# A fused linear-attention, Fourier and channel-mixing kernel: the gate computation in five parts issued in another order, zero matmuls placed elsewhere, Fourier tiles spread over more blocks

## The reference

```python
# stage 1, attention with a complex decay per token and channel
mag = np.sqrt(a_re * a_re + a_im * a_im)
scale = np.minimum(mag, 0.999) / (mag + 1e-06)
a_re_n, a_im_n = (a_re * scale, a_im * scale)
for t in range(S):
    new_re = ar * S_re - ai * S_im
    new_im = ar * S_im + ai * S_re
    kv = np.einsum('bhd,bhe->bhde', k[:, :, t], v[:, :, t])
    S_re, S_im = (new_re + kv, new_im)
    y[:, :, t] = np.einsum('bhd,bhde->bhe', q[:, :, t], S_re)
# stage 2
X = np.fft.fft(np.fft.fft(x, axis=1), axis=2)
u = x + np.real(X)
...
ch = np.maximum(un @ w_ch1, 0.0) @ w_ch2      # un is u, normalised by rows
return (u + ch)
# stage 3: token mixing and another two-layer product of the same sizes
```

## Time and profile before

| | us |
|---|---|
| runs | 1070.27, 1048.11, 1056.67 |
| median | 1056.67 |
| the profiled execution, own time | 1050.42 |
| its span (first to last instruction) | 1048.4 |
| PE busy | 982.1 (94%) |
| DVE busy | 514.9 (49%) |
| ACT busy | 357.8 (34%) |

### The profile page before, as it was taken

One profiled execution on the slowest core, in us unless ns is written; L12 is line 12 of the kernel. 1 busy time (PEld: TensorE's weight loads), 2 busy tenths in 40 slices (PEclk: granted clock), 3 DMA queues, 4 the chain that ended last, 5 costly groups with the idle time before them and its releaser, 6 DMA issues.

```text
span 1048.4 us, 15600 instructions
## 1 busy us (share of the span) xinstructions
PE 982.1 (94%) x6154; PEld 951.2 (91%) x6154; DVE 514.9 (49%) x940; ACT 357.8 (34%) x532; POOL 16.4 (2%) x12
## 2 busy tenths in 40 slices
PE   0389999999999999999999999999999999999997
PEld 0268889889899899999999999999999999999997
DVE  5888699999855654234324222542223214223220
ACT  7676666676531520220221221431213102121120
POOL 0000000000000000000000000030000000000000
PEclk9789899998999999999999999999999999999999
DMA  6689977986776064021021010010001001000000
GB/s 208 197 232 263 254 220 190 235 244 154 191 206 239 16 243 171 16 75 45 24 66 45 30 61 23 16 54 16 8 23 45 23 15 53 23 0 23 9 16 26
DMA packets 96745, 104.75 MB, mean 100 GB/s; under 512 B 13104, under 2 KB 90288, under 8 KB 96688
## 3 DMA queue, kind: packets, MB, share of 16 engines
q1 hardware_dynamic: 96688, 104.00, 33.6%
HBM read 70.86 MB, written 33.11 MB: 99 GB/s over the span
## 4 chain that ended last, share of the span: by engine, by line
PE 81%; DVE 8%; ACT 7%; issue 2%; DMA 0%; SPq 0%; DVEq 0%; ACTq 0%
PE bank L233 21%; PE bank L235 21%; PE bank L234 21%; PE bank L1173 3%; PE bank L1191 2%; DVE n_area L942 2%; PE bank L1189 2%; PE bank L1234 2%; PE bank L1250 2%; PE bank L1252 2%; PE bank L1202 2%; PE bank L1258 2%; PE bank L243 1%; DVE n_area L947 1%; DVE n_area L930 1%
## 5 line engine op out<-in xcount | busy, mean ns | idle before, releaser
L121 ACT ACTIVATE hh<-bank 128x384 fp32r<-128x384 f32 x192 | 94.5, 492 | 375.0 <-PE bank L235 375.0
L209 DVE SCALAR_TENSOR_TENSOR hl<-bank,hh 128x384 fp32r<-128x384 f32 x192 | 107.0, 557 | 195.6 <-ACT hh L121 195.6
L233 PE MATMUL bank<-w2h,hh 128*128 128x384 f32 x576 | 193.3, 336 | 0.0
L233 PE MATMUL bank<-nTh,w1h 128*128 128x384 f32 x576 | 193.0, 335 | 0.0
L235 PE MATMUL bank<-w2h,hl 128*128 128x384 f32 x576 | 192.5, 334 | 0.0
L234 PE MATMUL bank<-w2l,hh 128*128 128x384 f32 x576 | 192.5, 334 | 0.0
L235 PE MATMUL bank<-nTh,w1l 128*128 128x384 f32 x576 | 192.5, 334 | 0.0
L234 PE MATMUL bank<-nTl,w1h 128*128 128x384 f32 x576 | 192.4, 334 | 0.0
L233 PEld LDWEIGHTS bank<-nTh,w1h 128*128 128x128 f32 x576 | 108.1, 188 | 0.4 <-issue 0.2
L234 PEld LDWEIGHTS bank<-w2l,hh 128*128 128x128 f32 x576 | 108.2, 188 | 0.0
L234 PEld LDWEIGHTS bank<-nTl,w1h 128*128 128x128 f32 x576 | 108.1, 188 | 0.0
(11 more groups left out here) (156 smaller groups left out, 1294.1 us busy)
## 6 DMA issues: line engine op xcount, KB each, us to landing
w_area<-k_turn SPq DMA_DIRECT2D x24, 384.0 KB, 4.8
w_area<-q_turn SPq DMA_DIRECT2D x24, 384.0 KB, 6.1
q_turn<-w_raw SPq DMA_DIRECT2D x30, 192.0 KB, 3.0
k_turn<-n_area SPq DMA_DIRECT2D x24, 192.0 KB, 2.6
k_turn<-w_flat SPq DMA_DIRECT2D x24, 192.0 KB, 2.7
u_scratch<-h_area SPq DMA_DIRECT2D x24, 192.0 KB, 6.4
w_raw<-in_moe_w_ch SPq DMA_DIRECT2D x2, 2304.0 KB, 12.4
x_flat<-u_scratch SPq DMA_DIRECT2D x4, 1152.0 KB, 10.0
```

The costliest lines, as they stand in the source:

```text
L121: self.nc.scalar.activation(self.hh[:, m, :], self.mm_bank[(g * (KF + TPG) + m) % 2][:, 0:TG], ACT.Relu).then_inc(self.h_high, 1)
L209: self.nc.vector.scalar_tensor_tensor(out=self.hl[:, m, :], in0=self.mm_bank[(g * (KF + TPG) + m) % 2][:, 0:TG], scalar=0.0, in1=self.hh[: ...
L233: self.nc.tensor.matmul(out, lh, rh, start=(n == 0), stop=False)
```

## The change

- **Parts p0 to p4 are written out by hand**, interleaved with blocks 0 to 5 on ACT and DVE; the loop starts at block 6. `logs` is cut into `bounded` and `sums`, `magnitudes` loses its Abs to `moduli`, and `phases` is `half_turns`, `wrapped` per chunk, and `carried`. Counters `factored`, `summed`, `ended` and `qk_scaled` replace places in the running count of each part, so that the steps may stand in another order.
- **DVE issues `masked(0)` ahead of `phases(p2)`**, and `phases(p3)` is cut around `masked(3)`. ACT issues `keys_turned(0)` ahead of `inverses`, `arctangents` and `factors` of p2. There are six more table loads.
- **Zero matmuls**: 16, 2, 10, 1, 1, 8, 6, 5 in blocks 0 to 7, none in 12 and 18; 55 in all (60 before).
- **Fourier part**: `middle`, the width transforms and their evacuations move from j=1 to j=2. Tiles 0, 1 go to j=3, tile 2 to j=4, tile 3 to j=5, tiles 4 and 5 to j=0 and 1 of the batch after. For the last-but-one batch, tiles 4 and 5 run after block 23, in two other PSUM banks.
- **SP's queue**: block 0's products and `decay_back(p0)` go ahead of `decay_out(p1)`; `load_gates(p3)` follows at once, `load_qk(p3)` at the end of the opening.

```diff
 def transformed_at(...)
-            return {2: [0], 3: [1, 2], 4: [3, 4], 5: [5]}.get(j, [])
+            b, j = divmod(m, NCH)
+            n = b - 2 if j < 2 else b - 1
+            return [(n, i) for i in {3: [0, 1], 4: [2], 5: [3], 0: [4], 1: [5]}.get(j, []) if n >= 0]

         def added_at(m):
-            b, j = divmod(m, NCH)
-            n = b - 2 if j == 0 else b - 1
-            return [(n, i) for i in {3: [0], 4: [1, 2], 5: [3, 4], 0: [5]}.get(j, []) if n >= 0]
+            return transformed_at(m - 1) if m else []
...
 scalar engine, loop over blocks
-                if b and j == 1:
+                if j == 2:
                     middle(b - 1)
                     for n in range(KD):
                         widths(b - 1, n)
...
 vector engine, ahead of the loop
+            tangents(p2)
+            sums(p2)
+            dve.wait_ge(tables_in, 2 * 16)
+            masked(0)
+            advance_state(0)
+            squared(p3)
+            phases(p2)
+            masked(1)
...
+            advance_state(2)
+            half_turns(p3)
+            wrapped(p3, 0)
+            masked(3)
+            wrapped(p3, 1)
+            wrapped(p3, 2)
+            carried(p3)
...
 vector engine, after block 23
-            add_transform(B - 2, 5)
+            add_transform(B - 2, 3)
...
             fold_sequence(B - 1)
+            add_transform(B - 2, 4, st_bank)
+            add_transform(B - 2, 5, y_bank)
...
 tensor engine
             ahead = 3
+            WARM = [16, 2, 10, 1, 1, 8, 6, 5]
...
-                if m < NCH:
-                    keep_busy(5)
...
-                if b and j == 1:
+                if b and j == 2:
                     middle(b - 1)
                     for n in range(KD):
                         width_transform(b - 1, n)
-                if b:
-                    for n in transformed_at(j):
-                        sequence_transform(b - 1, n)
+                for n, i in transformed_at(m):
+                    sequence_transform(n, i)
                 if m:
                     turn_y(m - 1)
-                if b and j == 0:
-                    if b > 1:
-                        pe.wait_ge(b_added, (b - 1) * NT - 1)
-                    keep_busy(8)
+                if m < len(WARM):
+                    keep_busy(WARM[m])
```

More of the change, by code:

```diff
@@ L605, in _ @@
                         load_gates(p)
-                    if p.n > 2 and p.first == m + 6:
+                    if p.n > 3 and p.first == m + 6:
                         load_qk(p)
@@ L630, in _ @@
                 store_u(n, i)
-            store_u(B - 2, 5)
+            for i in range(3, NT):
+                store_u(B - 2, i)
             for i in range(NT):
@@ L778, in _ @@
             logarithm_tables()
[L779 removed]
+            p0, p1, p2, p3, p4 = parts[0:5]
             squares(p0)
+            magnitudes(p0)
+            moduli(p0)
             squares(p1)
[L782 removed]
+            inverses(p0)
             magnitudes(p1)
[L784 removed]
+            moduli(p1)
             factors(p0)
             inverses(p1)
[L787 removed]
             angle_tables()
@@ L792, in _ @@
             squares(p2)
+            logarithm_tables()
+            factors(p1)
+            magnitudes(p2)
+            moduli(p2)
+            angle_tables()
             sines(p1)
+            keys_turned(0)
             logarithm_tables()
-            magnitudes(p2)
             inverses(p2)
+            squares(p3)
+            angle_tables()
+            arctangents(p2)
+            logarithm_tables()
             factors(p2)
+            magnitudes(p3)
+            keys_turned(1)
+            evacuate_y(0)
             angle_tables()
-            for m in range(NM):
+            sines(p2)
+            y_turned(0)
+            keys_turned(2)
+            moduli(p3)
+            evacuate_y(1)
+            logarithm_tables()
+            inverses(p3)
+            angle_tables()
+            y_turned(1)
+            arctangents(p3)
+            keys_turned(3)
+            logarithm_tables()
+            factors(p3)
+            evacuate_y(2)
+            angle_tables()
+            y_turned(2)
+            squares(p4)
+            keys_turned(4)
+            evacuate_y(3)
+            sines(p3)
+            y_turned(3)
+            logarithm_tables()
+            magnitudes(p4)
+            moduli(p4)
+            evacuate_y(4)
+            y_turned(4)
+            inverses(p4)
+            factors(p4)
+            angle_tables()
+            for m in range(NCH, NM):
                 b, j = divmod(m, NCH)
@@ L925, in phases, with half_turns @@
+                V.tensor_tensor(k, k, t1_b[s][:, :, T], ALU.mult).then_inc(qk_scaled[s], 1)
             def phases(p):
-                s, n = p.s, vec0[p.n]
-                re, im = re_b[p.r], im_b[p.r]
+                half_turns(p)
+                for i in range(p.chunks):
+                    wrapped(p, i)
+                carried(p)
+            def half_turns(p):
+                s = p.s
+                im = im_b[p.r]
                 T = slice(0, p.T)
-                dve.wait_ge(act_step[s], act0[p.n] + 13)
+                dve.wait_ge(act_step[s], act0[p.n] + 11)
@@ L948, in phases @@
-                dve.wait_ge(vec_step[s], n + 9 + 3 * p.chunks)
+                T = slice(i * CT, (i + 1) * CT)
+                offset = slice(first + i * CT, first + (i + 1) * CT)
+                dve.wait_ge(vec_step[s], n + 5 + 3 * i)
+                for g in range(3):
+                    if i:
+                        start = t3_b[s][:, g, i * CT - 1:i * CT]
+                    else:
+                        start = carry[:, 1 - s, g:g + 1] if p.j0 else 0.0
+                    last = V.tensor_tensor_scan(t3_b[s][:, g, T], t3_b[s][:, g, T], t4[:, g, offset], start, ALU.add, ALU.add)
```

203 lines of the change are left out of this document (116 added, 87 removed).

## The result

The changed kernel takes 1061.53 us (median of 20 runs, 1054.66 to 1063.3), the kernel before 1058.2 (20 runs, 1048.11 to 1070.27): a ratio of 1.0056, with a 95% interval of 1.0035 to 1.0076. The forecast was 1050, a little faster. The profiled execution has a span of 1060.5 us.

A forecast was written before the change was run, and what follows sets the result against it. DVE and PE were taken as near full up to 353.16 us, PE setting the pace from masked(18). Terms -6.8 + 4.6 - 0.7 + 2.0 = -0.9 us on 1050.42 gave 1049.5, stated as 1050; range 1044 to 1056, 60%.

The forecast's parts named there:

- What bounds the kernel: Everything is decided in the first 353.16 us: DVE and PE near full, PE setting the pace from masked(18) on.
- The seventh stage: From 353.16 us to the end: 695.2 us, PE busy for 99% on products the change does not touch.
- The opening: Up to masked(6): reordered steps start products at 24.2 us and masked(0) at 46.1, filling DVE's waits: -6.8 us.
- M6: Start of masked(6), Mm being the start of masked(m): forecast at 129.2 us, from 136.04 before.
- named as a bound: At masked(3): a low clock over block 2's ten zero matmuls adds 6.7 us, about 5 reaching DVE; opening gain then -2.
- Batch 1: masked(6) to masked(12): widths ahead of `turn_y(7)` delay arctangents(p5); 78.7 us, +4.6 to 74.11.
- M9 - M8: From masked(8) to masked(9): 22.9 us instead of 16.94, with DVE idle some 8 us.
- The first rival: Blocks 8 and 14: the widths do not hold up the angles, -13.5 us in all, 1037 us; chance 15%.
- Batch 2: masked(12) to masked(18): removing zero matmuls gives back little; 75.9 us, -0.7 to 76.62.
- Batch 3: masked(18) to the last batch's first width transform: PE sets the pace with seven tiles instead of six, +2.0 us.
- The base: The whole kernel: the sum started from the profiled 1050.42 us, called a fast execution against the median of 1056.67.
- The rival of the clock: Blocks 2, 7, 13 and over the widths: low-clock stretches cost 3 to 5 us each, 1065 us; chance 20%.

The follow-up runs named there:

- kernel with four of them: Only the new opening on the kernel before, with 4 instead of 10 zero matmuls in block 2: 1044.86 us, once more 1050.54 us.
- before without late zeros: The kernel before without the eight zero matmuls in blocks 12 and 18, nothing else changed: 1062.6 us, ratio 1.0054.
- the kernel with the angles first: The changed kernel with `arctangents` of the next part ahead of `middle` and widths on ACT in blocks 8 and 14: 1064.55 us, ratio 1.0063.
- the Fourier part alone: The kernel before with only the new Fourier places and no zero matmuls in blocks 12 and 18: 1071.19 us, ratio 1.0108.
- one tile in block 9: The changed kernel with arctangents ahead of widths, eight zero matmuls in blocks 12 and 18, and one tile instead of two in block 9: 1056.59 us.
- zeros back: The changed kernel with eight zero matmuls again in blocks 12 and 18, into another PSUM bank: 1055.51 us, ratio 1.0007.
- angles first with zeros: The changed kernel with arctangents ahead of the width transforms and eight zero matmuls in blocks 12 and 18: 1063.71 us, ratio 1.0057.

## Why the prediction was wrong

Point by point, in the order of its sum.

**What bounds the kernel: right.** The seventh stage did not move (695.71 for 695.2 us).

**The opening: mechanism right, size too large.** The products start at 24.21 us (forecast 24.2) and `masked(0)` at 46.03 (46.1). M6 comes at 132.16, not 129.2: -3.9 for the -6.8 forecast. Of the missing 3 us, 2.2 are at `masked(3)`, where DVE waits 6.46 us and not 4.3. The ten zero matmuls ahead of it took 8.79 us, not 6.7, for they began within the stretch at the lower level from 73 to 80, behind a wait of PE of 3.69 us; this was named as a bound. The kernel with four of them has M6 at 129.5 and 128.4. In runs the opening is worth 0.4 to 0.5%, 4 to 6 us (by the medians 7 to 9). A part of that may lie in the reference: both profiles of before have a low stretch ahead of M6 (102 to 113, and 89 to 100), and the one of before without late zeros has none and M6 at 131.6. How much of the opening's gain is order and how much clock is not settled.

**Batch 1: right, with misses that cancel.** 79.10 us for 78.7. M8 is 12.7 us behind M7 (forecast 10.8; the five zero matmuls took 5.88 us at the lower level for 3.3), and M9 - M8 is 21.8 (22.9), with the wait of 7.25 us for the angles where some 8 were expected: 1.9 us too little and 1.1 too much. The first rival, that the widths hold nobody up, is out. The claim that the ACT order is the cause was half of it: the kernel with the angles first has the shorter M9 - M8 and the same M10. `middle`, three widths and two tiles ahead of two successive `turn_y` are the load, and any of ACT's steps behind `y_turned` inherits it.

**Batch 2: the step that failed.** Forecast 75.9 us, measured 84.92. The sentence was that the late zero matmuls are issued while PE would wait anyway, "So their removal gives back little", and the sum took nothing for them. The first half holds: in their place PE waits for DVE, 4.85 us in the kernel before without them. The conclusion does not. Removed, they cost 0.5% by the ratios, about 5 us, alone as well as within the change, and 3 and 6 us by the medians; with the angles first they made no difference. With them back in the changed kernel batch 2 takes 78.8 us.

What they were worth is the clock behind them. Without them PE comes to a wait, and the clock falls in it or within 2.5 us of its end: 4.85 us for `masked(12)` in the kernel before without them and 3.62 us with the angles first; 2.31 us for `evacuate_y(12)` in the changed kernel, the Fourier part alone and the kernel without zero matmuls in block 7. These stretches last 13 to 18 us and, except in the kernel with the angles first, reach `middle` or the width transforms. In the three profiles of the new places with zero matmuls in blocks 12 and 18, PE has no wait above 1 us in blocks 12, 13 and 18; in two of them no low stretch begins there, and in the third (one tile in block 9) one of ten us from 226, with PE busy. Why a short wait should do this in block 13 is not shown beyond this agreement of the profiles.

The mechanism stood in the forecast as a rival, with 3 to 5 us per stretch on the path and 20%. The case against it was that PE is idle for less than 4.5 us at a time. That was no argument: the row at 252 had already shown the clock falling with no such wait at all, and a wait of 2.31 us stood ahead of the costliest fall of the changed kernel.

By the two profiles the zero matmuls explain 6.1 of the 9.0 us by which batch 2 was missed. The other 2.9 stand also in the profile with them back, 78.8 us for 75.9. There M15 - M14 is 20.3 us, where 18.7 were forecast, with 5.82 us of waiting for the angles ahead of `phases(p7)`, where 4 were expected. In the changed kernel this wait is 10.69 us and M15 - M14 is 25.9, because `middle` and widths (7.50 us for 6.17) and what stands ahead of them ran at the lower level.

**Batch 3: right in its number, perhaps by luck.** 68.61 us for 68.4. The low stretch from 284 to 299 reaches 3 us into this stage, and the two profiles that have no low stretch near or behind M18 (zeros back, and angles first with zeros) have 67.0. So up to 1.6 us may be the clock's, and the forecast's +2.0 too much by as much; no run separates the two.

**The base.** The sum was made from 1050.42 us, the profiled execution, and stated as 1050. The median of before is 1058.2, 7.8 higher. The forecast said that the profiled execution was a fast one and took no step from there. The mean granted clock was 0.978 in it, 0.974 in the repeated profile, and 0.971 in the median of the runs of before; from this one can estimate 46, 54 and 61 us at the lower level, so that a typical execution has one or two low stretches more than the first profile. The priced ones took 2.0 to 4.9 us each. Carried over to the median and with 5.4 us for the late zero matmuls, the forecast's -0.9 would read 1058.2 - 0.9 + 5.4 = 1062.7; measured were 1061.53. That this is near is no proof of the terms, for the opening's was too large by 2 us or so and the intervals are 2 to 5 us wide to either side.

**The rival of the clock** had put stretches in blocks 2, 7 and 13 and over the widths, and 1065. The profile has them at 73 (block 2), 141 (blocks 6 and 7), 226 (block 13, and on over the widths of block 14), and besides at 35, 110, 199 and 284 us, where it had named none; the median is 3.5 us below its time. This rival came nearer than the forecast. The page that was weighed against it (the Trainium skill, "TensorE: Matmul & The Clock Gate", HAM oscillation: waits between bursts put the clock back) would have made it the rule. The falls at 73, 110, 141 and 226 us of the changed kernel, in or behind 3.69, 5.36, 3.83 and 2.31 us in which PE is idle, go with that page, and so do those at the waits of 4.85 and 5.95 us in before without late zeros. The ten to eleven us from 252 in before and the 14 us from 199 in the changed kernel, with no wait above 0.6 us shortly ahead of them and PE busy throughout, are not explained by it.

## What to carry to other kernels

Filler work in a wait has a price only where it ends after what the engine waits for, and a worth in the clock of what comes behind it: cost its removal by what the next burst would take at the lower level, look for the waits that its removal opens further on, and vary its length, for here four were better than none, and no worse than ten. When a block of work is moved on one engine, add up what then stands ahead of each hand-over to another; reordering the receiver's list moves such a wait by a block and does not remove it. And before a sum is set against a median, count in the profile what can differ from one execution to the next (here the low stretches), and add its usual number to the base.

## What the runs showed of the hardware

- TensorE's granted clock fell in two ways. It fell in or just behind idle times of PE of 2.3 to 6 us, and then stayed at the lower level for 7 to 18 us (110, 141 and 226 us in the changed kernel; 208 and 287 in before without late zeros). It also fell for ten to fourteen us with PE busy throughout and no wait above 0.6 us just ahead (252 in before, 199 in the changed kernel). All of this was beside the attention blocks with their matmuls of 48 to 128 columns; in the last stage (695 us, mostly of 384 columns) the mean is 1.00.
- A stretch of the second kind, of ten to eleven us, cost 4.1 us where it began at 158 or 161 us (stage 78.2 for 74.1), 2.5 where it began between 252 and 257, and 4.9 at 325, behind M18. One that ended at M12 or M18 left its own stage as it was and cost 2.0 and 3.0 us in the two blocks behind it.
- In which block the isolated stretches come differs between executions of one kernel: 102 and 252 in one profile of before, 89, 198 and 253 in another; none between 116 and 344 us in one of the kernel with four zero matmuls, three in the next.
